# Change-over from attention and hand-over between two MLP blocks: new orders on all engines, three weight pairs per pass in the second block

## The reference

```python
# attention, 2 x 8 heads, 768 tokens, 64 wide
mask = q_assign[:, :, :, None] == k_assign[:, :, None, :]   # nearest of 16 centroids
attn = softmax(where(mask, q @ k.T / 8, -1e9)); x = attn @ v  # -> x: 1536 x 512
# block 1: w_in 512 x 2048, w_out 2048 x 512
h = x @ w_in
g = where(h >= 1, h, where(h <= -1, 0, (h + 1) ** 2 / 4)); x = g @ w_out
# block 2: w_gate, w_val 512 x 1536, w_out 1536 x 512
xn = x / sqrt(mean(x * x) + 1e-6) * rms_g
out = (silu(xn @ w_gate) * (xn @ w_val)) @ w_out
```

## Time and profile before

| | |
|---|---|
| runs | 873.32, 877.00, 877.12 us, median 877.0 |
| the profiled execution | 878.67 us, its span 876.8 us |
| busy share of the span | PE 94%, DVE 76%, ACT 55%, POOL 49% |
| TensorE's mean granted clock | 0.977 of full speed |
| attention | 0 to 288 us of the span |
| block 1, steps 0 to 23, and block 2, steps 24 to 59 | 288 to 873.6 us |

### The profile page before, as it was taken

How to read it: one execution, slowest core, us unless ns; L and a number is a source line. 1 busy time by engine, 2 the same in 40 slices (tenths; PEclk the granted TensorE clock), 3 DMA queues, 4 the chain that set the end, 5 groups by cost and what they waited for, 6 DMA issues and landing times. The chain is left out here.

```text
span 876.8 us, 15461 instructions
## 1 busy us (share of the span) xinstructions
PE 820.3 (94%) x5341; PEld 746.3 (85%) x5341; DVE 667.4 (76%) x1228; ACT 485.0 (55%) x867; POOL 433.6 (49%) x374
## 2 busy tenths in 40 slices
PE   4999999999999769999999999887999999999998
PEld 4898898898887658999999888776999999999997
DVE  4798898898887396565665668897777878787776
ACT  3778888788787357666566557654432222222221
POOL 0134533323365991561560667999581909183400
PEclk9899999999999889999999999998899999999999
DMA  6766456456331100110110010020110101020012
GB/s 139 168 160 147 110 131 139 108 135 138 87 77 43 45 13 1 49 49 1 49 49 25 25 49 20 17 61 1 37 37 25 49 25 49 3 72 1 25 49 96
DMA packets 65503, 54.88 MB, mean 63 GB/s; under 512 B 30112, under 2 KB 52640, under 8 KB 65440
## 3 DMA queue, kind: packets, MB, share of 16 engines
q1 hardware_dynamic: 65440, 54.06, 24.7%
HBM read 27.30 MB, written 3.15 MB: 35 GB/s over the span
## 5 line engine op out<-in xcount | busy, mean ns | idle before, releaser
L706 PE MATMUL ps<-th,wh 128*128 128x256 f32 x840 | 243.5, 290 | 23.9 <-ACT snap L884 9.0
L706 PE MATMUL ps<-tl,wh 128*128 128x256 f32 x840 | 241.3, 287 | 0.0
L706 PE MATMUL ps<-th,wl 128*128 128x256 f32 x840 | 241.2, 287 | 0.0
L706 PEld LDWEIGHTS ps<-th,wh 128*128 128x128 f32 x840 | 164.4, 196 | 30.4 <-issue 10.3
L706 PEld LDWEIGHTS ps<-tl,wh 128*128 128x128 f32 x840 | 164.7, 196 | 2.3
L706 PEld LDWEIGHTS ps<-th,wl 128*128 128x128 f32 x840 | 164.7, 196 | 0.0
L1052 DVE TENSOR_SCALAR_CACHE_REDUCE sf<-ps 128x768 f32<-128x768 f32 x96 | 91.3, 951 | 29.1 <-PE ps L552 27.4
L1333 POOL TENSOR_TENSOR wl<-wraw,wh 128x448 fp32r<-128x448 f32 x80 | 101.7, 1302 | 1.6
L803 ACT ACTIVATE pbuf<-sf,minn 128x768 f32<-128x768 f32 x96 | 89.7, 935 | 22.1 <-DVE sf L1052 21.8
L793 ACT ACTIVATE pth<-ps 128x512 fp32r<-128x512 f32 x144 | 84.5, 589 | 30.1 <-PE ps L576 19.1
L1061 DVE TENSOR_TENSOR ptl<-ps,pth 128x512 fp32r<-128x512 f32 x144 | 95.6, 682 | 5.2 <-ACT pth L793 5.1
(11 more groups left out here) (132 smaller groups left out, 1833.0 us busy)
## 6 DMA issues: line engine op xcount, KB each, us to landing
q<-atile SPq DMA_DIRECT2D x32, 192.0 KB, 3.3
k<-atile SPq DMA_DIRECT2D x32, 192.0 KB, 3.5
o1raw<-in_moe_w_out SPq DMA_DIRECT2D x8, 512.0 KB, 3.6
nat<-in_q SPq DMA_DIRECT2D x16, 192.0 KB, 3.8
nat<-in_k SPq DMA_DIRECT2D x16, 192.0 KB, 4.0
q<-btile SPq DMA_DIRECT2D x16, 192.0 KB, 3.2
k<-btile SPq DMA_DIRECT2D x16, 192.0 KB, 4.0
vnat<-in_v SPq DMA_DIRECT2D x16, 192.0 KB, 3.7
```

The costliest lines, as they stand in the source:

```text
L706: last = pe.matmul(dst[:, 0:HC], a[w][:, j, kt, :], b[c][:, j, kt, :], start=(opened and kt == 0 and i == 0), stop=(kt == KH - 1 and i == ...
```

## The change

In the last heads of attention, `fill_out(0)`, `t_sum(0)`, the first `t_hi` and `t_lo` come two heads earlier. The load of pair 1 is issued at the beginning of the last head's block; POOL makes its sums and high part there too, and its low part later in the block. After attention, the first two steps are written out by hand on ACT and DVE, and PE does up(0), up(1), down(0), down(1), up(2), up(3), down(2).

In the hand-over, `rms_g` is multiplied in by ACT right behind each square, and no longer by POOL. The widening on DVE (L1238) is gone: PE reads the reciprocal with a broadcast. All tables have new step numbers, and `t_hi` and `t_lo` are spread in smaller pieces. ACT takes all four tiles of the first group of block 2. For chunk 0, `spread_inverse` comes after down(22) instead of before it, and `inverse_out` after the step's high parts.

Block 2 has groups of three pairs: 4 groups of 9 steps in place of 6 groups of 6. Its second weights have six buffers in place of four. The first weights still have three buffers, and each group needs three.

```diff
-        o2h = [place(f"o2h{i}", [P, DM], F32R, O00, 2 * i * DM * 4) for i in range(4)]
...
+        O2H = [O00 + 2 * i * DM * 4 for i in range(4)] + [G0 + (4 * i + 1) * CH * 4 for i in range(2)]
...
-        LOOP0, LOOP1 = 4, NH - 4
+        LOOP0, LOOP1 = 4, NH - 6
...
-                 [(1, [NP1 + 2 * b, NP1 + 2 * b + 1]) for b in range(NP2 // 2)]
+                 [(1, [NP1 + 3 * b + i for i in range(3)]) for b in range(NP2 // 3)]
...
-        SQUARES_AT = (20, 22, 24)
-        SUMS_AT = (21, 24, 26)
-        NORM_AT = (22, 25, 27)
-        SPREAD_AT = (23, 26, 28)
-        SPLIT_AT = (22, 24, 26)
+        SQUARES_AT = (21, 23, 25)
+        SUMS_AT = (22, 25, 27)
+        NORM_AT = (23, 26, 28)
+        SPREAD_AT = (23, 27, 30)
+        SPLIT_AT = {(22, 0): (3, 0, 2), (22, 1): (3, 2, 1), (23, 0): (3, 3, 2), (23, 1): (3, 5, 2),
...
             def blk(n, u, fixed, pair):
+                if fixed == NH - 1:
+                    sp.wait_ge(scores_done, NT * NH)
+                    load_up(1)
...
-            load_up(NP1 + 2)
-            for q in range(NP1 + 2, NP1 + NP2, 2):
-                load_up(q + 1)
-                if q + 2 < NP1 + NP2:
-                    load_up(q + 2)
-                    load_out2(q + 2)
-                    load_out2(q + 3)
+            for q in range(NP1 + 3, NP1 + NP2, 3):
+                for i in range(3):
+                    load_up(q + i)
+                if q + 3 < NP1 + NP2:
+                    for i in range(3):
+                        load_out2(q + 3 + i)
...
-                if s in SPREAD_AT:
+                if s in SPREAD_AT[1:]:
                     spread_inverse(SPREAD_AT.index(s), s)
-                if s:
+                if s == 1:
+                    down(0)
+                    down(1)
+                elif s > 2:
                     down(s - 1)
+                if s == SPREAD_AT[0]:
+                    spread_inverse(0, s)
...
+                act.activation(sq[c][:, SQ_AT[m], :], x, ACT.Square).then_inc(squared, 1)
+                act.wait_ge(squared, KT * c + m + 1)
+                act.activation(x, x, ACT.Copy, scale=rmsg[:, m:m + 1]).then_inc(x_scaled, 1)
...
-                dve.wait_ge(rms_inverse, c + 1)
-                dve.tensor_scalar(z[c][:, :].rearrange("p (m i) -> p m i", m=TPC),
-                                  zt[c][:, :].unsqueeze(2).to_broadcast([P, TPC, P]), 1.0, None, ALU.mult).then_inc(inverse_widened, 1)
...
-                if fixed == NH - 1:
-                    for i in range(4, PROD):
-                        first_t_lo(i)
-                    fill_up(1)
+                if fixed == NH - 1:
+                    low_up(1)
...
+                if fixed == NH - 1:
+                    sum_up(1)
+                    high_up(1)
...
             prepare(0)
             fill_up(NP1 + 1)
+            fill_up(NP1 + 2)
+            fill_out(NP1)
             prepare(1)
-            fill_out(NP1)
             fill_out(NP1 + 1)
+            fill_out(NP1 + 2)
             prepare(2)
```

More of the change, by code:

```diff
@@ L330, in build @@
         up_loaded = [sem(f"up_loaded{i}") for i in range(3)]
-        out_loaded = [sem(f"out_loaded{i}") for i in range(4)]
+        out_loaded = [sem(f"out_loaded{i}") for i in range(6)]
         up_summed = sem("up_summed")
@@ L951, in take_y @@
             def take_y(s, m):
[L952 removed]
+                if not closes(s) or not first_block(s):
                     return
@@ L961, in take_y, with t_hi_at @@
                     act.activation(x, bank(Y[m]), ACT.Copy).then_inc(y_done[m], 1)
-            for s in range(NS):
+            def t_hi_at(s, slot):
+                if (s, slot) in HIGH_AT:
+                    t_hi(*HIGH_AT[s, slot])
+            snap(0)
+            copy_corner(0)
+            bend(0, 0)
+            snap(1)
+            hidden_hi(0, 0)
+            bend(0, 1)
+            copy_corner(1)
+            hidden_hi(0, 1)
+            bend(1, 0)
+            t_hi(1, 0, 1)
+            hidden_hi(1, 0)
+            bend(1, 1)
+            t_hi(1, 1, 2)
+            hidden_hi(1, 1)
+            t_hi(1, 3, 4)
+            for s in range(2, NS):
                 mlp = STEPS[s][0]
                 snap(s)
[L966 to L971, removed]
                 if s == 3:
                     t_hi(2, 3, 4)
-                if s - 1 in SQUARES_AT:
-                    squares(SQUARES_AT.index(s - 1), 2)
-                    squares(SQUARES_AT.index(s - 1), 3)
                 if s in SUMS_AT[1:]:
                     sums_hi(SUMS_AT.index(s))
-                if s in SPLIT_AT:
-                    t_hi(3 + SPLIT_AT.index(s), 0, 4)
-                if s - 1 in SPLIT_AT:
-                    t_hi(3 + SPLIT_AT.index(s - 1), 4, 3)
+                t_hi_at(s, 0)
+                if s in SQUARES_AT:
+                    squares(SQUARES_AT.index(s), 0)
+                    squares(SQUARES_AT.index(s), 1)
                 copy_corner(s)
-                if s == 1:
-                    hidden_hi(0, 1)
-                    t_hi(1, 0, 7)
-                if s == 2:
-                    hidden_hi(1, 1)
                 if mlp == 0:
@@ L1004, in _ @@
                         rms(NORM_AT.index(s))
+                    t_hi_at(s, 1)
                     hidden_hi(s, 0)
-                take_y(s - 1, 2)
-                take_y(s - 1, 3)
+                    for m in range(KT):
+                        take_y(s - 1, m)
+                if s == SPREAD_AT[0]:
+                    inverse_out(0)
                 if s == 2:
                     t_hi(2, 0, 3)
+                if s in SQUARES_AT:
+                    squares(SQUARES_AT.index(s), 2)
+                    squares(SQUARES_AT.index(s), 3)
                 if s == SUMS_AT[0]:
                     sums_hi(0)
-                if s in SQUARES_AT:
-                    squares(SQUARES_AT.index(s), 0)
-                    squares(SQUARES_AT.index(s), 1)
         @block.vector
@@ L1193, in take_y @@
             def take_y(s, m):
-                if s < 0 or not closes(s) or (first_block(s) and m >= 2):
+                if s < 0 or not closes(s) or (first_block(s) and (STEPS[s][0] or m >= 2)):
                     return
@@ L1300, in _ @@
                     sums_lo(0)
+            for m in range(KT):
+                take_y(NS - 1, m)
         @block.gpsimd
@@ L1482, in _ @@
             blocks(pool, blk)
-            for k in range(4):
-                t_sum(1, k)
+            t_sum(1, 0)
+            t_sum(1, 1)
             fill_out(1)
+            t_sum(1, 2)
+            t_sum(1, 3)
+            pool.wait_ge(hidden_low, HALVES[2])
             for k in range(4):
```

175 lines of the change are left out of this document (86 added, 89 removed).

## The result

The changed kernel takes **884.29 us** (median of 8 runs, 882.33 to 886.56), the kernel before 879.1 us beside it (8 runs, 873.32 to 880.57): ratio 1.0069, 95% interval 1.0043 to 1.0095. It is slower by 0.7%. The execution that was profiled took 883.33 us, its span is 881.5 us, the mean granted clock 0.977, as before.

A forecast was written before the change was run, and what follows sets the result against it. PE, busy for 94% of the span, was taken as the bound: its work plus its waits. 876.8 - 4.4 - 1.2 + 12.0 = 883.2 us of span, giving a median of 883.4; 883.5 us likeliest, range 864 to 894.

The forecast's parts named there:

- the change-over: From attention into the first steps, up to U4: wait before up(1) goes, new waits come; -4.4 us, between -9 and +2.
- the three pairs: Block 2: third fill late by 3.2 us at three group transitions, plus 0.8 us of clock each; +12.0 us, 0 to +15.
- the hand-over: From U20 to U32: 17.2 us of waits and 5.5 us of clock against 23.9 lost before; -1.2 us, between -12 and +6.
- half of its price: Block 2's three transitions: 0.8 us each taken for the half clock behind a wait, where the bound was 1.7.
- The wait inside up(3): Change-over: up(3)'s fifth product waits about 6.5 us for the snap, and 1.4 more behind DVE's first sums.
- the four waits of 4.5 us: Change-over: down(0) and down(1) wait, half by half, for bends and low parts, 0.8 to 1.5 us each, 4.5 in all.
- U0: Start of up(0) after attention: expected at 288.5, 0.5 us later, because the last head's reciprocals come later.
- up(24): Hand-over: up(24) waits for `inverse_out`, which ends at 568.4 while PE is ready at 564.0; 4.4 us.
- up(23)'s share: Hand-over, step 23: waits behind `t_hi`, squares and scalings, and for DVE behind `sums_lo`; 3.4 us.
- snap(28): Hand-over: snap(28) stands behind transpose, silu's table load and four takes on ACT; 3.5 us.
- The faster rival: Hand-over runs clean as POOL's missing scalings free DVE: hand-over -12, change-over -6, transitions +9; 868 us, chance 0.28.
- The rival of no difference: Fills overlap PE's wait at 9.9 us on average, 4 us lost in all; 875.5 us, or terms cancel otherwise; chance 0.22.

The follow-up runs named there:

- early snap: snap(3) moved ahead of step 2's remaining work on ACT, its sums ahead on DVE, tried on three kernels: 865.0, 864.8 and 865.1 us.
- runs with one part alone: The kernel before with only the change-over part, 868.9 us, and the kernel before with only groups of three pairs, 901.8 us.
- three pieces first: Changed kernel, but in later groups of block 2 up waits for three low-part pieces at its start, the fourth before its sixth product: 880.0 us.
- three pairs alone: Kernel before with groups of three pairs, six second-weight buffers and the change's order of loads and fills; tables and scaling as before: 901.8 us.
- scaling on GpSimd: Changed kernel with the scaling of x put back on POOL: 893.9 us.
- by piece: Changed kernel with block 2's later low parts awaited piece by piece at the products that read them, here also with snap(3) moved ahead: 864.8 us.
- change-over alone: Kernel before with only the change's last heads, first steps and PE order, here also with snap(3) moved ahead: 865.0 us.

## Why the prediction was right, and where it was not

The forecast was 883.5 us, slower; 884.29 us came. The sign and the mechanism behind it were right. That the number is so near is in part luck: the forecast stood on a median of 877.0 us for the kernel before, which was 879.1 with more runs, so that 6.4 us more were forecast and 5.2 came; and the change-over came out 3.9 us better than forecast, the three pairs 2.8 us worse. The 0.7% (0.4 to 1.0%) is also only just over the 0.5% from which the prediction calls a kernel slower. (Two sums in its text are off by a little and change nothing: the waits of the hand-over add up to 17.1 us, and 876.8 + 4 - 5.6 is 875.2.) Step by step:

- **Three pairs, +12.0 forecast, +14.8 measured.** The mechanism and the places are those forecast: U35, U44 and U53 wait for POOL's low parts for 3.00, 3.12 and 3.14 us, against 3.2. In the second transition the third pair was forecast ready 42.1 us behind U39; it was 42.0 (701.32 to 743.34). The start was 0.9 us sooner than counted, the fills 10.5, 10.8 and 11.5 us. The term that was mis-sized is the clock: I took half of its price, 0.8 us; all three stretches came, at 1.7. The term stayed within its bounds of 0 and +15, at the upper end.
- **Change-over, -4.4 forecast, -8.3 measured at U4.** The wait before up(1) went. The fill started at 275.26 and ended at 287.40, earlier than the 290.7 of the working. The wait inside up(3) was 6.00 us and 1.3 more behind DVE's sums, forecast 6.5 and 1.4, and the reason given for it is shown by the early snap. Of the four waits of 4.5 us before it, three came, 4.05 us, and the 0.9 us in up(2) did not come. The clock was at half for 13.6 us, not 8, which took back some of it. What was missed is U0: forecast 0.5 later, in fact 2.7 us earlier. More than half of that is no effect of the change. Near the beginning, where both kernels run the same code, the profiled execution of before has 6.8 us at half clock and that of after has none (before, then after, granted clock 0.50 and 1.00):

```profile
28.60:35.40 6.80, 6.80 (x28) 6.67 (x28) 4.17 (x9) 3.59 (x7) 1.52 (x3) 0.50 0.48 114
28.60:35.40 6.80, 5.75 (x40) 5.12 (x39) 4.74 (x12) 4.61 (x10) 2.09 (x3) 1.00 0.63 150
```

Three kernels with the change's last heads have that stretch too, and their U0 is at 286.7 to 287.0, 0.9 to 1.2 us before the 287.94 of before; the seven that don't have it are at 284.7 to 285.6. What the change itself gave shows in PE's waits in the last heads: for ACT's copy of the reciprocals (`rsb`) 0.5 us in place of 1.0, and for the last head's widened reciprocals from POOL none in place of 0.5, where the forecast had put these 0.5 us later.
- **Hand-over, -1.2 forecast, -1.5 measured**, by two errors that cancel. PE waited 13.1 us, not 17.2: up(24) 2.9 in place of 4.4, up(23)'s share 3.7 (forecast 3.4), snap(28) 2.2 in place of 3.5. Half clock was 17 us, not 11. The chain to up(24) ran as forecast: `inverse_out` ended at 562.93 and up(24) began at 563.14. It had stood behind a high part that waited 3.75 us for DVE.

```profile
561.82 0.63 ACT L927 ACTIVATE gh<-hid 128x512 fp32r<-128x512 f32 x1 [3.75 <-DVE hid L1200]
562.35 0.58 ACT L966 ACTIVATE z<-ps 128x512 f32<-128x512 f32 x1
```

- **What the sum could not see.** I set the hand-over against that of before and costed three pairs by block 2 alone. The runs with one part alone say that they are tied by POOL's queue: three pairs without the new hand-over cost 24 us, not 12. The scaling's move pays for most of that: without it the changed kernel is 9.6 us slower. The sum came right because both were made; each term as the price of its own edit was not.
- **The faster rival** needed the hand-over at -12, from DVE's operations falling from 1.2 to 0.7 us. They fell by little. The 19 low parts between 505 and 650 us, before and after (busy us, mean ns of one):

```profile
L1190 DVE TENSOR_TENSOR gl<-hid,gh 128x512 fp32r<-128x512 f32 x19 | 20.5, 1093 | 1.1 <-ACT gh L914 0.7
```

```profile
L1217 DVE TENSOR_TENSOR gl<-hid,gh 128x512 fp32r<-128x512 f32 x19 | 18.8, 1001 | 4.5 <-ACT gh L927 4.2
```

Nor was this the scalings' doing. With them back on POOL, the 17 low parts from U20 to U32 took 1024 ns on average, in the changed kernel 1027; and in the kernels with two pairs they went from 980 to 1250 ns when the scalings left POOL. What counts is what POOL does beside the one operation. In the twelve traces that were kept, 563 of these low parts met no work of POOL and took 0.68 to 0.70 us each; 101 had, for most of their time, only POOL's low parts of weights beside them and took 1.12 us on average, up to 1.63; of DVE's low parts of both kinds (`gl` and `tl`) 14 had only a scaling beside them, and took 0.77 on average. Of the two in the earlier trace rows that took 2.38 us, the first, begun beside the end of a scaling, took 0.68, and the second, beside POOL's sums, 1.61. The Trainium skill (SBUF — State Buffer, "Who interferes with whom") has VectorE blocked by GpSimd on a shared read port: the traces agree for two-input work of POOL, 1.12 against 0.69 us, but not that the scalings, with one input tile each, were much time for DVE, as the prediction took it.
- **The rival of no difference** had fills of 9.9 us that overlap the wait. They took 10.5 to 11.5 us; they didn't get faster while PE and DVE stood.

Open: why the clock is at half near the beginning of some executions and not of others, and what the 3.09 us wait for DVE in up(23) would give if DVE's low parts were put elsewhere; neither was tried.

## What to carry to other kernels

Buffers that come free late make an idle engine a late one: count from when a buffer is released, through issue and fills in a row, to when the work is due, before making a pass as wide as all the buffers there are. Then have the consumer wait for each piece at the product that reads it; here that alone was worth some 12 us. And judge moving an operation from one engine to another by which engine is waited for in that schedule: moving the same 12 scalings was worth 9 to 10 us in one and cost 3 to 5 us in the other.

## What the runs showed of the hardware

- A wait of PE can cost more than itself. In block 2, where PE had been busy with no wait over 0.8 us for 25 us and more, twelve waits for POOL stand in four traces (changed kernel 3.00, 3.12, 3.14 us; three pieces first 2.42, 3.05, 2.10; three pairs alone 3.20, 3.36, 3.36; scaling on GpSimd 2.60, 3.13, 3.27). At the end of eleven of them, the shortest and the longest included, the clock is at 1.2 GHz for 3.4 us, some 1.7 us lost each; at the end of the one of 2.60 us it is not. It isn't at any wait of 0.5 to 0.8 us there either.
- The same wait can fall on either side: behind the 2.21 us in up(28) of the changed kernel the clock stayed full, while behind the same wait in the kernel with groups of 3, 2, 2, 2, 3 it was at half for 3.4 us. At the `down` behind up(3) with snap(3) early, 1.98 us (by piece) had none and 2.02 us (change-over alone) 3.4 us.
- The mean granted clock was 0.988 in the kernel with 865.0 us, 0.977 before. Within the span the clock is at half for 20.5 us in the one trace and for 41.0 in the other; 6.8 of the 20.5 us between them are the stretch near the beginning, in code that the change doesn't touch. Of the 15.0 us that the span is shorter, 8.4 are PE's busy time (811.9 against 820.3), since the same matmuls ran for less of it at half clock, the stretch near the beginning included.
- A DVE operation of one shape has no fixed price: the low part of a 128x512 tile took 0.69 us with POOL idle and up to 1.6 us beside POOL's two-input work of the same kind.
